# Shorter routing, and tile 0 in front of two weight products, in an attention and two-MoE kernel

## What is computed

```python
# first mixture
logits = x @ phi
slot_input = softmax(logits, axis=0).T @ x          # 32 slots
slot_out[e] = np.maximum(slot_input[e] @ w1[e], 0.0) @ w2[e]
x = softmax(logits, axis=1) @ slot_out
# second mixture
noisy = x @ w_gate + np.log1p(np.exp(x @ w_noise)) * noise
top2 = the two largest of 8; weights = softmax over the two
for e in range(E):
    for k in range(2):
        mask = top2[:, k] == e
        h = np.maximum(x[mask] @ w1[e], 0.0)
        out[mask] += top2_w[mask, k, None] * (h @ w2[e])
```

## Time and profile before

| what | us |
|---|---|
| median of 3 runs | 549.07 (546.41 to 551.51) |
| the profiled execution, its own time | 547.3 |
| its span, first to last instruction | 545.6 |
| TensorE busy | 496.7 (91% of the span) |
| VectorE, ScalarE, GpSimd busy | 277.1, 185.3, 257.9 |
| mean granted TensorE clock | 0.969 of full |

### The profile page before, as it was taken

One profiled execution on the slowest core, in us unless ns is written; L12 is line 12 of the kernel. 1 busy time (PEld: TensorE's weight loads), 2 busy tenths in 40 slices (PEclk: granted clock), 3 DMA queues, 4 the chain that ended last, 5 costly groups with the idle time before them and its releaser, 6 DMA issues.

```text
span 545.6 us, 13537 instructions
## 1 busy us (share of the span) xinstructions
PE 496.7 (91%) x4845; PEld 294.6 (54%) x4846; DVE 277.1 (51%) x449; ACT 185.3 (34%) x345; POOL 257.9 (47%) x216
## 2 busy tenths in 40 slices
PE   4898989997977568799999999999999999999995
PEld 4686777873476344345545455454554545545452
DVE  1775757565411698573564645454646242332422
ACT  0121222222000835773645544536352222322210
POOL 1222221212000016455686868686887766656543
PEclk9999999998997688899999999999999999999998
DMA  7999999988999999415554452123232343333410
GB/s 274 358 353 417 373 379 389 336 337 305 420 424 426 403 414 380 165 51 193 188 191 136 125 179 55 30 52 52 36 59 43 47 57 44 47 50 41 55 24 1
DMA packets 32358, 107.91 MB, mean 198 GB/s; under 512 B 11567, under 2 KB 12831, under 8 KB 27840
## 3 DMA queue, kind: packets, MB, share of 16 engines
q1 hardware_dynamic: 18144, 92.89, 44.0%
q0 software_dynamic: 14176, 14.49, 14.7%
HBM read 93.87 MB, written 29.43 MB: 226 GB/s over the span
## 4 chain that ended last, share of the span: by engine, by line
PE 81%; DMA 7%; DVE 6%; issue 3%; ACT 1%; POOL 1%; SPq 0%; DVEq 0%; POOLq 0%
PE ps L988 51%; PE ps L971 5%; PE ps L655 4%; PE ps L719 4%; DMA late_w1a<-chunks 3%; PE ps L861 3%; PE ps L839 3%; DMA w_region<-chunks 3%; PE ps L695 2%; PE ps L709 2%; PE ps L730 1%; PE ps L669 1%; DMA rec_region<-records,idx 1%; PE ps L751 1%; PE ps L922 1%
## 5 line engine op out<-in xcount | busy, mean ns | idle before, releaser
L988 PE MATMUL ps<-w_region,s_region 128*128 (+1 forms) x1320 | 294.9, 380 | 1.1 <-ACT s_region L1177 1.1
L988 PEld LDWEIGHTS ps<-w_region,s_region 128*128 128x128 f16 x1320 | 127.1, 98 | 144.8 <-issue 2.6
L1607 DVE SCALAR_TENSOR_TENSOR s_region<-ps,s_region 128x1024 f16<-128x1024 f32 x55 | 67.4, 1225 | 147.0 <-ACT s_region L1177 147.0
L1177 ACT ACTIVATE s_region<-ps 128x1024 f16<-128x1024 f32 x55 | 56.3, 1024 | 182.3 <-PE ps L971 182.3
L606 POOL DMA_INDIRECT out<-s_region,rec_region x41 | 55.8, 1361 | 52.7 <-DVE s_region L1636 49.9
L612 POOL DMA_INDIRECT out<-s_region,rec_region x42 | 67.9, 1616 | 15.1 <-issue 12.2
L600 POOL DMA_INDIRECT rec_region<-records,idx x55 | 62.0, 1127 | 24.8 <-issue 16.5
L546 POOL TENSOR_TENSOR s_region<-w_region,s_region 128x512 f32<-128x512 f32 x14 | 14.8, 1058 | 51.4 <-PE ps L730 26.7
L971 PEld LDWEIGHTS ps<-s_region,sw_region 128*128 (+1 forms) x440 | 29.7, 99 | 15.7 <-issue 3.0
L1636 DVE TENSOR_SCALAR s_region<-ps,rec_region,y_scale 128x512 f32<-128x512 f32 x42 | 33.8, 805 | 6.5 <-PE ps L988 4.6
L971 PE MATMUL ps<-s_region,sw_region 128*128 128x128 f16 x440 | 34.5, 222 | 1.9 <-ACT sw_region L1130 1.9
(11 more groups left out here) (248 smaller groups left out, 568.8 us busy)
## 6 DMA issues: line engine op xcount, KB each, us to landing
w_region<-moe_w SPq DMA_DIRECT2D x11, 2048.0 KB, 8.6
w_region<-moe_w SPq DMA_DIRECT2D x15, 1024.0 KB, 9.8
w_region<-chunks SPq DMA_DIRECT2D x26, 512.0 KB, 7.3
w_region<-moe_w SPq DMA_DIRECT2D x24, 512.0 KB, 17.2
s_region<-moe_w SPq DMA_DIRECT2D x4, 2048.0 KB, 15.1
sw_region<-chunks SPq DMA_DIRECT2D x12, 512.0 KB, 7.7
late_w1a<-chunks SPq DMA_DIRECT2D x8, 512.0 KB, 8.6
s_region<-moe_w SPq DMA_DIRECT2D x2, 1024.0 KB, 10.9
```

What stands on the lines that cost most here:

```text
L988: last = nc.tensor.matmul(bank[6 + r], h[:, r, f, :], w2b_parts[:, bass.ds(o, 1), part, f, :].rearrange("p e m -> p (e m)"), start=(first ...
L1177: nc.scalar.activation(h_hi[:, r, :, :].rearrange("p c t -> p (c t)").rearrange("p (a n) -> p a n", a=2), ps[:, 2 + 2 * r:4 + 2 * r, :], A ...
L1607: nc.vector.scalar_tensor_tensor(out=h_lo[:, r, :, :].rearrange("p c t -> p (c t)").rearrange("p (a n) -> p a n", a=2), in0=ps[:, 2 + 2 * ...
```

## The change

- Routing: the slot outputs are turned in two halves and copied by VectorE and ScalarE together; the four copies into `g_diag` are one product with a mask; the counts use FP16 operands, and the triangle holds -1 so that the inclusive scan plus its product gives the place directly; the tile counts come from an integer shift; the two products and reductions of the places are one each over both choices.
- VectorE: the order of the experts (`order_ready`) is computed ahead of the first scales and the index, in place of between `sw_low(3)` and `w2b_low(0)`. The tile codes take fewer operations.
- ScalarE: the first half sum of w2b(0) stands ahead of the gates' exponential.
- TensorE: product 4 behind the sort, then the spreads of experts 0 to 3, product 5, turn and first layer of tile 0, turn of tile 1, 8 matmuls of tile 0's second layer, product 6, 8 more, product 7, spreads of experts 4 and 5, tile 0's last 8 matmuls, spreads of 6 and 7, the first layers of tiles 1 and 2, all of tile 1's second layer and 16 matmuls of tile 2's; tile 3's first layer; the loop from tile 3.
- Expert 7 has a scale group of its own. Units 9, 11, 14 and 15 are copied by VectorE, the others by ScalarE.
- w2b of order 1: the half sums are split around the staging of tiles 2 and 3 on ScalarE; GpSimd's all-reduce stands behind the write and add of tile 0; VectorE scales and splits it between `h_low(2)` and `keep_y(1)`. Sums of order 2 come one tile later (`SUMS`).

The diff, cut to its core:

```diff
+    SUMS = {o: FIRST[o] + (o == EARLY + 1) for o in FIRST}
...
-        SW_GROUPS = ((0, 4), (4, E))
+        SW_GROUPS = ((0, 4), (4, E - 1), (E - 1, E))
+        SW_BANKS = (6, 1, 0, 7, 6, 1, 0, 6, 1, 0, 7, 1, 0, 7, 1, 0)
+        SW_BY_DVE = (9, 11, 14, 15)
...
+        def turned_slots(first, last):
+
+            return (bank[4 if first == 0 else 3][:, 0:(last - first) * SL].rearrange("p (c s) -> p c s", s=SL).unsqueeze(2)
+                    .to_broadcast([P, last - first, REP, SL]))
...
             sw_all_sum(*SW_GROUPS[1])
+            sw_all_sum(*SW_GROUPS[2])
             for i in range(DEPTH + 2, 2 * DEPTH + 3):
                 fetch_records(i)
-            w2b_all_sum(EARLY)
...
+                if i == 0:
+                    w2b_all_sum(EARLY)
                 for o in FIRST:
-                    if i == FIRST[o] - 1:
+                    if i == SUMS[o] - 1:
                         w2b_all_sum(o)
...
-            nc.tensor.transpose(bank[4][:, 0:P], slot_out_4, ident[:, :]).then_inc(slot_out_turned, 1)
-            pe.wait_ge(slot_out_ready, 1)
+            pe.wait_ge(c_t_ready, 1)
+            for n in range(2):
+                part = slice(n * P // 2, (n + 1) * P // 2)
+                last = nc.tensor.transpose(bank[4 - n][:, 0:P // 2], slot_out_4[part, :], ident[part, part])
+            last.then_inc(slot_out_turned, 1)
+            pe.wait_ge(slot_out_ready, 2)
...
-            nc.tensor.matmul(bank[0][:, 0:E * NT], before[:, :], chosen, start=True, stop=True)
-            nc.tensor.matmul(bank[0][:, 256:256 + E * NT], ones[:, :], chosen, start=True,
-                             stop=True).then_inc(ranks_done, 1)
-            sw_product(1)
-            for e in range(2, 5):
+            nc.tensor.matmul(bank[0][:, 256:256 + E * NT], ones_h[:, :], chosen, start=True, stop=True)
+            nc.tensor.matmul(bank[0][:, 0:E * NT], not_before[:, :], chosen, start=True, stop=True).then_inc(ranks_done, 1)
+            for e in range(1, 4):
                 sw_product(e)
...
                 sort_rows(part)
+            sw_product(4)
+            pe.wait_ge(idx_ready, 1)
+            for e in range(4):
+                sw_spread_parts(e)
             sw_product(5)
-            pe.wait_ge(sw_lo_ready, 4)
-            sw_spread_parts(0)
-            sw_spread_parts(1)
-            sw_product(6)
-            sw_spread_parts(2)
-            sw_spread_parts(3)
...
+            pe.wait_ge(*sw_kept(3))
             turn_c(0, 0, 7)
-            sw_product(7)
...
             hidden_b(0, 0, 0)
-            turn_c(1, 1, 1)
-            out_b(0, 0, 0, True)
-            pe.wait_ge(ct_ready, 2)
-            for e in range(4, E):
-                pe.wait_ge(sw_lo_ready, e + 1)
-                sw_spread_parts(e)
+            turn_c(1, 1, 7)
+            pe.wait_ge(*sw_kept(7))
+            pe.wait_ge(w2b_hi_ready, 2)
+            pe.wait_ge(h_hi_ready, 1)
+            first_rows(0, range(FC))
+            sw_product(6)
+            pe.wait_ge(w2b_lo_ready, 1)
+            first_rows(1, range(FC))
+            sw_product(7)
+            sw_spread_parts(4)
+            sw_spread_parts(5)
+            out_b(0, 0, 0, False)
+            sw_spread_parts(6)
+            sw_spread_parts(7)
             pe.wait_ge(tile_code_ready, 1)
-            pe.wait_ge(*sw_kept(11))
+            pe.wait_ge(*sw_kept(13))
             pe.wait_ge(*sw_kept(15))
...
+            hidden_b(1, 1, expert_of(code))
+            turn_c(2, 0, 0)
+            hidden_b(2, 0, expert_of(code_of(2)))
+            turn_c(3, 1, 1)
+            o = order_of(code)
+            out_b(1, 1, o, True)
+            out_b(1, 1, o, False)
...
+            out_b(2, 0, order_of(pe.snap(kept, min_val=0, max_val=E * E - 1)), True)
...
-            with pe.Fori(0, (RT - 3) // 2) as k:
+            with pe.Fori(1, (RT - 3) // 2) as k:
...
+            act.wait_ge(slot_out_turned, 1)
+            nc.scalar.activation(slot_out_t[:, DC // 2:DC, :, :], turned_slots(DC // 2, DC),
+                                 ACT.Copy).then_inc(slot_out_ready, 1)
+            w2b_sum_part(0, 0, junk_slots[0])
             act.wait_ge(gate_done, 1)
...
+            sw_sums(4)
+            for unit in range(E):
+                sw_keep(unit)
             sw_sums(5)
...
             stage_c(0, 0, rec_arrival(0))
-            for unit in range(4, E):
-                sw_keep(unit)
             keep_ct(0, 0)
             stage_c(1, 1, rec_arrival(1))
-            sw_sums(7)
             h_high(0, 0)
             keep_ct(1, 1)
+            sw_sums(6)
+            act.wait_ge(sw_scale_ready, 2)
+            for e in range(4, 7):
+                sw_high(e)
+            sw_sums(7)
+            sw_keep(8)
+            sw_keep(10)
+            act.wait_ge(sw_scale_ready, 3)
+            sw_high(7)
+            sw_keep(12)
+            sw_keep(13)
+            w2b_sum_part(EARLY, 0, junk)
             stage_c(2, 0, rec_arrival(2))
...
             h_high(1, 1)
             keep_ct(2, 0)
+            stage_c(3, 1, rec_arrival(3))
+            h_high(2, 0)
+            keep_ct(3, 1)
+            w2b_sum_part(EARLY, 1, junk)
             w2b_high(EARLY)
...
-            for n in range(REP):
-                part = slice(n * SL, (n + 1) * SL)
-                last = nc.vector.tensor_copy(g_diag[part, n, :], bank[6][part, 256:256 + 2 * E])
-            last.then_inc(g_ready, 1)
+            nc.vector.tensor_tensor(g_diag[:, :, :], bank[6][:, 256:256 + 2 * E].unsqueeze(1).to_broadcast([P, REP, 2 * E]),
+                                    quarter[:, :].unsqueeze(2).to_broadcast([P, REP, 2 * E]), ALU.mult).then_inc(g_ready, 1)
...
+            link(nc.vector.tensor_tensor_scan(out=incl.rearrange(flat), data0=reset.rearrange(flat),
+                                              data1=bank[0][:, 256:256 + E * NT], initial=0.0, op0=ALU.mult, op1=ALU.add))
+            tiles_i = per_e[:, 0, :].bitcast(I32)
+            link(nc.vector.tensor_tensor(slots, incl, bank[0][:, 0:E * NT].rearrange("p (e t) -> p e t", e=E), ALU.add))
+            link(nc.vector.tensor_scalar(tiles_i, incl[:, :, NT - 1], float(P - 1), None, ALU.add))
+            link(nc.vector.tensor_scalar(tiles_i, tiles_i, P.bit_length() - 1, None, ALU.logical_shift_right))
+            link(nc.vector.tensor_scalar(per_e[:, 1, :], tiles_i, 1, None, ALU.max))
...
+            link(nc.vector.scalar_tensor_tensor(out=slot_no, in0=over_t(per_e[:, 3, :]), scalar=float(P), in1=slots,
+                                                op0=ALU.mult, op1=ALU.add))
...
+            link(nc.vector.tensor_tensor(slots_both, slot_no.unsqueeze(1).to_broadcast([P, 2, E, NT]), ones_both, ALU.mult))
+            link(nc.vector.tensor_reduce(pos_f[:, :, :], slots_both.rearrange("p n e t -> p n t e"), AX_X, ALU.add))
...
+            h_low(0, 0)
             sw_scales(1)
-            h_low(0, 0)
-            for e in range(4, E):
+            for e in range(4, 7):
                 sw_low(e)
-            for unit in range(E, E + 4):
-                sw_keep(unit)
+            sw_keep(9)
+            sw_keep(11)
+            sw_scales(2)
+            sw_low(7)
+            sw_keep(14)
+            sw_keep(15)
...
-            w2b_scale_by_sum(EARLY)
-            scale_y(EARLY)
...
+            low_keep(0, 0, None)
+            h_low(2, 0)
+            w2b_scale_by_sum(EARLY)
+            dve.wait_ge(order_ready, 1)
+            scale_y(EARLY)
+            w2b_low(EARLY)
+            keep_y(1, 1, None)
+            for i in range(2, UNROLLED):
```

More of the change, by code:

```diff
@@ L185, in build_program @@
         ident_h = sb("ident_h", [P, P], F16)
-        before = sb("before", [P, P], F32)
+        not_before = sb("not_before", [P, P], F16)
+        ones_h = sb("ones_h", [P, P], F16)
         ones = sb("ones", [P, P], F32)
@@ L362, in build_program @@
         block = ctx.enter_context(nc.Block())
-        SW_GROUPS = ((0, 4), (4, E))
+        SW_GROUPS = ((0, 4), (4, E - 1), (E - 1, E))
+        SW_BANKS = (6, 1, 0, 7, 6, 1, 0, 6, 1, 0, 7, 1, 0, 7, 1, 0)
+        SW_BY_DVE = (9, 11, 14, 15)
+        SW_BY_ACT = tuple(u for u in range(2 * E) if u not in SW_BY_DVE)
         W2B_SUMS = 2
         FINE = 3
-        sw_out = [ps[:, 2 + e // 2, e % 2 * QF:(e % 2 + 1) * QF] for e in range(E)]
+        sw_out = [ps[:, 2 + e // 2, e % 2 * QF:(e % 2 + 1) * QF] for e in range(E - 1)] + [ps[:, 2, 0:QF]]
         SC = ((0, 1), (2, 3))
@@ L902, in sw_spread_parts @@
             def sw_spread_parts(e):
+                pe.wait_ge(sw_lo_ready, e + 1)
                 for half in range(2):
                     unit = 2 * e + half
-                    if unit >= 3 and unit not in (8, 9, 10):
-                        pe.wait_ge(*sw_kept(unit - 3))
+                    before_it = [u for u in range(unit) if SW_BANKS[u] == SW_BANKS[unit]]
+                    if unit == 10:
+                        pe.wait_ge(ct_ready, 2)
+                    elif before_it:
+                        pe.wait_ge(*sw_kept(before_it[-1]))
```

(27 more changed lines are left out.)

133 lines of the change are left out of this document (54 added, 79 removed).

## The result

The changed kernel takes 554.91 us, the median of 4 runs (551.52 to 557.69); the kernel before took 548.54 in the same comparison. The ratio is 1.0123, with a 95% interval of 1.0083 to 1.0163: slower by 1.2%, where 549.5 and no change were forecast. Its profiled execution took 556.63 us, its span 554.6, so the traces stand 9.0 us apart in span and the medians 6.4.

A forecast was written before the change was run, and what follows sets the result against it. The chain was read as 81% TensorE, with tile 4's first layer as the mark. Terms of -5.3, +6.05 and -0.25 summed to +0.5 us: median 549.5, no change, 8-in-10 range 545.0 to 552.5.

The forecast's parts named there:

- Routing: From the slot outputs to the index: shortened routing makes the index ready at 203.35 against 206.40, 3.05 us sooner.
- rival c: Records' write replaces the index as what holds the fetches; each us above 9.4 costs one, 551.5 at 11.4; chance 0.08.
- The second fetch: GpSimd's fetch held by w2b_low to 208.2; tile 1's records land at 213.1, tile 0's second layer starts at 214.4.
- Work in front of tile 1: From tile 0's second layer to tile 1's first layer: 13.7 us plus 1.5 for low clock, against 9.15 before.
- From tile 1 to tile 4: Between their first layers: 18.4 us against 18.65 before, with 1.3 us of TensorE's to spare hiding most low clock.
- The chain of w2b(1): From tile 1's first layer through all-reduce, scale and split to keep_y(1): 14.9 us, which tile 3's out_b waits for.
- The loop: From tile 4 on: no waits, 5.68 us a tile, so the end moves by as much as tile 4's start.
- (b): Rival on w2b(1)'s chain: first write's 2.88 us is the price of being first; +3.3, 552.4 us; chance 0.10.
- (a): Rival at tile 0: the second fetch doesn't hold h_high(0); -2.3, 546.8 us; chance 0.27.
- (d): Rival: with (a), the clock stays up too, or routing gives 3.5; -4, 545.1 us; chance 0.10.

The follow-up runs named there:

- e6: The changed kernel with keep_y(1) ahead of w2b_low(1) on VectorE and the load of w2b order 3 held until h_high(5): 1.0025 of the kernel before.
- e1: The changed kernel with the load of w2b order 3 held until h_high(5) in place of h_high(3): 548.14 us, 1.0015 of the kernel before.
- e9: e6 plus unread matmuls, nine behind the last spread and five ahead of tile 2's first layer: 1.0005 of the kernel before.
- e5: The changed kernel with VectorE's keep_y(1) ahead of w2b_low(1), the load of order 3 left as it is: 1.0054 of the kernel before.
- e7: e6 with the last eight matmuls of tile 0's second layer moved behind tile 2's turn: 1.0025 of the kernel before.
- e8: e6 with w2b_low(0) moved behind the tile codes on VectorE: 1.0042 of the kernel before.
- e2: The changed kernel with w2b(1)'s half sums moved behind keep_ct(1), its all-reduce and scale also earlier: 1.0149 of the kernel before.
- e4: The kernel before with the change's routing part alone, its order of products, spreads and tiles kept: 0.9984 of the kernel before.

## Why the prediction was wrong

- **Routing** was right: index at 203.29 for 203.35 (31.15 for 31.57 from the copy); the reduction of 384 columns took 1.08 for the 1.18 taken, and w2b_low(0) started at 204.96 for 204.95. The record write (rival c) set nothing.
- **The second fetch** was right in size: 2.47 us, 0.9 behind w2b_low's first half. Its price was not: ScalarE staged tile 1 at 213.23 without a wait, because the sixth product ran at half clock (3.60) and the sum came later still. e6 shows the wait of 1.68 that I had forecast, with the product at 1.93. One of the two comes last. Behind the index tile 0's second layer came 11.9 us later for the 11.05 forecast; it was 10.5 to 10.9 in e1, e6 and e9, where the product ran at full clock and the fetch held ScalarE, and 11.8 to 12.2 in e5, e7 and e8, at the low one. So the 215.21 for 214.4 is near by luck: another wait stood in the place of the forecast one. The lock that the Trainium skill describes ("SBUF — State Buffer", section "SBUF: two separate sides") is seen again, with a tail of 0.9 and not the 115 ns of its section "A bandwidth-pool intuition that's wrong".
- **Work in front of tile 1**: 16.0 us for the 15.2 forecast. The term was mis-sized at the clock: eight matmuls took 3.57, 1.84 over full clock, for the 1.5 taken, and the waits between products and spreads 0.5 more.
- **From tile 1 to tile 4**, 20.4 for 18.4. The step that failed here is "TensorE's own 1.3 us to spare there also hide most of a stretch at 1.2 GHz". The stretch is longer. The windows of after around it:

```profile
230.00:235.00 5.00, 2.34 (x18) 1.65 (x18) 1.55 (x5) 2.61 (x6) 1.59 (x2) 0.73 0.08 10
235.00:240.00 5.00, 4.84 (x15) 1.86 (x15) 2.46 (x6) 3.08 (x4) 3.03 (x3) 0.59 0.17 58
```

  TensorE was busy 2.34 of 5 us while it waited for stagings, and the granted clock fell to 0.59. The 40 matmuls took 10.70 for 8.64, and the first layers with their waits 4.0 for 2.8: 3.3 us, not the 1.3 that were to spare. The chain of w2b(1) itself ended at +16.4 for +14.9, of which 1.2 came in ahead of tile 0's write. Both came out nearly level, as e7's waits show, so neither alone gives the 2 us back.
- **The loop** is the largest error. "The diff leaves the loop's body alone. So the end moves by as much as the start of a tile once the loop runs without a wait" took it for granted that it would. The step behind it was "the weight stream runs beside it, and I leave its order as it is". The load of order 3 did keep its place, 0.8 us behind h_high(3) in both kernels; what moved against it is tile 1's write. The prediction had keep_y(1) late, behind w2b_low(1), and priced that for TensorE's out_b(3) alone; it didn't follow the write that keep_y(1) releases. Its issue went from 3.8 us ahead of the load to 0.4, and its time to landing from 2.8 us to 10.40. e1, e5 and e2 each part the two in another way, and the loop gives back 4.4 us; with e1 the whole is 1.0015. Nor is the body quite untouched: `SUMS` has the sums and the all-reduce of order 2 one tile later, behind one write and add more. In e1 the all-reduce keeps that place, and tile 7's turn still waits 0.28 us for ScalarE: tiles 4 to 7 take 17.5 for 17.0 of before. Half a us may be its price without a collision. With one it may be more: in after, the half sums of order 2 were done at 255.4, so in its old place, 1.0 us behind the start of tile 2's add (258.55), the all-reduce would have stood at about 259.6 for 262.78. That is an estimate from these rows, and its 3.2 us are as much as the turn's wait of 2.97. So the collision is needed for the loss, as e1 and e5 show; how much it would have cost with `SUMS` left alone is an open rival that no run tested.
- **Rivals.** (b) named a chain that did come late and the wrong cause: the first write took 1.03, not 2.88. (a) and (d) would have needed tile 1 sooner; even in e9, with the sixth product and tile 0 at full clock, the entry took it back.

So most of the 6.4 us of the medians goes when the collision does: e1 leaves 1.0 of them, e5 2.9. Why e5 leaves more by the medians than e1, when their traces end alike, stays open; their intervals overlap.

What the change sought is there in part. Taking tile 0 in front of two products escapes the landing that holds e4 (second layer 4.6 to 7.4 us sooner), but the spreads, all-reduces and stagings that came behind it give it all back by tile 1: 56.9 to 59.3 for 57.10 in every version that isn't slower still, but e9.

## What to carry to other kernels

Where a step is moved, list what its end releases, writes and loads alike, and look at what else starts at that moment: the weight stream can keep its order and its place while a write is moved into it. And follow what is queued behind that write, not only the engine that the step feeds. A scattered write with waiters in its queue should be issued ahead of a large load, or the load held back, as in e1 by two tiles. And before routing or any other front stage is shortened, look for the landing that ends last behind it: here 2.6 us on VectorE were worth nothing in front of it (e4).

## What the runs showed of the hardware

- A write of 128 rows of 2 KB, issued together with a 2 MB load, landed in 10.40 us; with no load in flight the median was 2.8 (e1, 225 to 250 us, six writes and adds), and the load took 9.8 for 8.0. The write landed 0.2 us behind the load (258.3 and 258.1). Writes issued 1.5 us into the flight of such a load did so too: 7.0 us and 0.3 behind it in before (the write at 245.77), 6.9 and 0.3 in e1 (257.36). The Trainium skill, "DMA: Bandwidth & Descriptors" (section "Issuing engines are not separate DMA queues"), says that transfers run on the same 16 DMA engines and interleave, whichever engine issued them. The trace agrees; that the small one would land no sooner than the large one I had not expected.
- GpSimd's indirect DMA is held by VectorE's FP32-to-FP16 operation on two SBUF operands: 2.47 and 1.96 us for 1.00, 2.89 in e5, and 4.52 in e8. There it started 0.95 us behind the start of the first half of w2b_low(0) (203.93 to 208.52) and ended 0.88 behind the second half: it was held through both. How far into the first half it starts doesn't decide this alone: in before, a fetch issued 1.2 us into the first half (210.13, half from 208.94) was let through between the two.
- The granted clock isn't the same in two executions of one order of work. Up to tile 0's second layer, e6, e7 and e9 have the same instructions. The sixth product took 1.93, 3.52 and 1.93 us, the first eight matmuls behind it 3.40, 3.39 and 1.89. One trace can't settle an edit that is worth 2 us of clock.
